# Diagonal blocks of a token ranking by six fused multiply-and-compare steps, and three pairs' late additions moved from TensorE to VectorE and GpSimd

## The reference, cut to what matters

```
ub = np.sum(np.maximum(q * k_min, q * k_max), axis=-1)      # a bound for each query and chunk
top_chunks = np.argsort(ub, axis=-1)[..., -top_k:]          # top_k = 6
scores = np.where(sel & causal, scale * q @ k.T, -1e9)
attn = exp(scores - max) / sum(exp(scores - max));  x = attn @ v
...
expert_idx = np.argmax(x @ w_gate, axis=1)
keep = np.argpartition(-gw, capacity)[:capacity]            # capacity = 80
out[tok_idx] = gate_w[tok_idx, None] * (np.maximum(x[tok_idx] @ w1[e], 0) @ w2[e])
```

## Time and profile before

| | us |
|---|---|
| median of 3 runs | 268.12 |
| lowest and highest run | 266.79, 274.02 |
| profiled execution | 266.53 |
| its span, first to last instruction | 264.8 |
| TensorE busy in the span | 256.2 |
| VectorE busy | 213.2 |
| GpSimd busy | 211.3 |
| ScalarE busy | 149.6 |

### The profile page before, as it was taken

How to read it: one execution, slowest core, us unless ns; L and a number is a source line. 1 busy time by engine, 2 the same in 40 slices (tenths; PEclk the granted TensorE clock), 3 DMA queues, 4 the chain that set the end, 5 groups by cost and what they waited for, 6 DMA issues and landing times.

```text
span 264.8 us, 9133 instructions
## 1 busy us (share of the span) xinstructions
PE 256.2 (97%) x3824; PEld 164.4 (62%) x3824; DVE 213.2 (81%) x582; ACT 149.6 (56%) x227; POOL 211.3 (80%) x280
## 2 busy tenths in 40 slices
PE   7799999999999999999999999999999999989993
PEld 7366566666666566666665666656665657676763
DVE  6886696778989988867889889899999998983332
ACT  2295656565667564647584546564856665873320
POOL 6068889998999899897989898979899971726872
PEclk9999999999999999999999999999999999999999
DMA  9989989999799989997999999999799996941782
GB/s 147 189 145 149 235 225 261 228 187 224 125 208 180 209 145 195 173 219 125 215 160 215 171 190 164 215 162 324 142 207 184 328 212 142 165 103 40 136 167 91
DMA packets 148616, 48.34 MB, mean 183 GB/s; under 512 B 131583, under 2 KB 138870, under 8 KB 148512
## 3 DMA queue, kind: packets, MB, share of 16 engines
q1 hardware_dynamic: 135504, 28.73, 54.1%
q0 software_dynamic: 9936, 18.64, 38.6%
q10 hardware_dynamic: 3136, 0.39, 1.0%
HBM read 57.03 MB, written 11.01 MB: 257 GB/s over the span
## 4 chain that ended last, share of the span: by engine, by line
PE 91%; DVE 3%; ACT 2%; DMA 1%; issue 1%; ACTq 1%; POOL 0%; DVEq 0%
PE OB L637 28%; PE SC L546 27%; PE SC L567 7%; PE OB L1395 4%; PE MM L673 4%; PE SC L1369 4%; PE MM L650 3%; PE OB L721 2%; PE MM L474 2%; PE SC L474 2%; PE MM L513 2%; DMA qn<-in_q_dram 1%; ACT EXB L576 1%; PE MM L712 1%; PE MM L982 1%
## 5 line engine op out<-in xcount | busy, mean ns | idle before, releaser
L576 ACT ACTIVATE EXB<-SC 128x1024 f32<-128x1024 f32 (+1 forms) x87 | 83.1, 966 | 35.6 <-PE SC L546 23.9
L602 POOL TENSOR_TENSOR ES<-ES,EXB 128x512 f32<-128x512 f32 (+1 forms) x81 | 84.4, 1044 | 5.1
L546 PE MATMUL SC<-qT,kT 64*128 64x512 f32 (+3 forms) x476 | 86.3, 464 | 0.1
L637 PE MATMUL OB<-EXB,vn 128*64 128x256 f32 (+3 forms) x704 | 72.9, 361 | 0.0
L637 PEld LDWEIGHTS OB<-EXB,vn 128*64 128x64 f32 x704 | 46.1, 137 | 24.0 <-issue 10.4
L546 PEld LDWEIGHTS SC<-qT,kT 64*128 64x128 f32 x476 | 39.2, 187 | 15.8 <-issue 11.5
L602 POOL TENSOR_TENSOR ES<-EXB 128x512 f32<-128x512 f32 (+1 forms) x29 | 45.3, 1561 | 2.4
L586 POOL TENSOR_SCALAR_AFFINE_SELECT EXB<-EXB 128x256 f32<-128x256 f32 x79 | 34.9, 452 | 5.0 <-ACT EXB L576 5.0
L645 ACT ACTIVATE oT<-OB 128x512 f32<-128x512 f32 (+1 forms) x32 | 15.7, 490 | 40.1 <-PE OB L637 40.1
L567 PE MATMUL SC<-unsT,ind 64*128 64x256 bf16 (+5 forms) x238 | 35.6, 295 | 0.1
L567 PEld LDWEIGHTS SC<-unsT,ind 64*128 64x128 bf16 x238 | 11.8, 95 | 15.9 <-issue 7.1
(11 more groups left out here) (270 smaller groups left out, 405.0 us busy)
## 6 DMA issues: line engine op xcount, KB each, us to landing
w1s<-in_moe_w_dram POOLq DMA_DIRECT2D x8, 1024.0 KB, 8.6
w2s<-in_moe_w_dram POOLq DMA_DIRECT2D x7, 1024.0 KB, 13.9
vn<-in_v_dram SPq DMA_DIRECT2D x32, 192.0 KB, 4.5
kn<-in_k_dram SPq DMA_DIRECT2D x62, 96.0 KB, 3.2
qn<-in_q_dram SPq DMA_DIRECT2D x62, 96.0 KB, 3.5
out_dram<-w1s SPq DMA_DIRECT2D x2, 1536.0 KB, 7.2
out_dram<-out_dram SPq DMA_DIRECT2D x2, 1536.0 KB, 9.8
x_rows<-xp SPq DMA_DIRECT2D x7, 384.0 KB, 3.9
```

The source lines that it names most:

```text
L546: op("pe", lambda: pe.matmul(o, kT[j][pr, ts(kt)], qT[j][pr, q0:q1], start=not flags and (not cols or cols[0] == 0), stop=bool(flags)), r= ...
L576: op("act", lambda: ac.activation(Ex(st, None, 0, W), src, ACTF.Exp, scale=SCALE), r=pk, w=[f"E{st}"])
L602: op(e, lambda: sy.queue[e].tensor_tensor(o, in0, in1, ALU.add), r=[f"E{s2}", f"E{first[0]}"] if first else [f"E{s2}"] + kt, w=kt)
L637: op("pe", lambda: pe.matmul(OB[pr, q0:q1], vn[s][:, kt, h, :], ex, start=(n == 0), stop=last), r=[f"vn{s}{h}", "ES0" if st is None else f ...
```

## The change

`direct` names no pair any more. So in pairs 5, 9 and 13 the eight products of line 668 are gone, VectorE makes the addition of line 608, and the second late addition is GpSimd's in pairs 5 and 9 and VectorE's (line 611) in pair 13. `rank_own` is gone, and `rank_diag` is six instructions, one per block, each of which multiplies the 128 by 128 triangle by the block's weights, one scalar for each partition, and compares the product with the block's part of G. Thirty small products are put ahead of TensorE's first ones, and of those 40 are left in place of 52; their results are not used. The instructions of the changed kernel have other line numbers: the fused ones stand in line 835, the comparisons in 842, the count in 973.

```diff
                 def direct(i):
-                    return mid(i) and i > NPB and i % NPB == 1
+                    return False
...
-                def rank_own(b):
-                    tq = bass.AP(triQ, 0, [[128, 128], [0, NT], [1, 128]])
-                    gb = bass.AP(gt6, 0, [[NT, 128], [1, NT], [0, 128]])
-                    op("dve", lambda: ve.tensor_tensor(T1v(b).rearrange("p (a b) -> p a b", a=NT), tq, gb, ALU.mult),
-                       r=["triQ", "gt6"], w=["T1"] + Ck(b, NT - 1))
-
                 def rank_diag(b):
-                    for j0, n in ((NT - 1, 1), (0, NT - 1)):
-                        o = Cs(b, j0, n, 0, 128)
-                        a = T1v(b)[:, j0 * 128:(j0 + n) * 128].rearrange("p (a b) -> p a b", a=n)
-                        g = G[:, S + j0 * 128:S + (j0 + n) * 128].rearrange("p (a b) -> p a b", a=n)
-                        op("dve", lambda: ve.tensor_tensor(o, a, g, ALU.is_ge), r=["T1", "grow"] + Ck(b, NT - 1),
-                           w=[f"D{jt}" for jt in range(j0, j0 + n)] + Ck(b, j0))
+                    for jt in range(NT):
+                        op("dve", lambda: ve.scalar_tensor_tensor(Cs(b, jt, 1, 0, 128)[:, 0, :], triQ[:], gt6[:, jt:jt + 1], G[:, S + jt * 128:S + (jt + 1) * 128],
+                                                                  ALU.mult, ALU.is_ge), r=["triQ", "gt6", "grow"], w=[f"D{jt}"] + Ck(b, jt))
...
-                warm(52, 152)
+                for n in range(30):
+                    c = n % 4 * 32
+                    op("pe", lambda: pe.matmul(SC[1][c:c + 32, 0:32], ident_f[:, 0:32], ident_f[:, 0:32], start=True, stop=True),
+                       r=["ident_f"], w=["SC1"], inc=False)
+                warm(40, 152)
...
-                    if live and kk == 0:
-                        rank_own(bb)
```

## The result

The changed kernel takes 282.01 us (median of 6 runs, 279.80 to 285.37) against 268.97 for the kernel before (median of 6, 266.79 to 274.02): a ratio of 1.049, 95% interval 1.042 to 1.056. The prediction had 276.0 and a range up to 277.8. So the sign was right, the loss of 13.0 us was half as large again as the 8.5 forecast, and the time is outside the range.

The account below looks back on a forecast made before the run. It took TensorE, busy 97% of the span, as the bound. Later count starts in pairs 6, 10 and 14 of 2.4 + 2.4 + 3.7 = 8.5 us, on a base of 267.5, gave 276.0, range 270.5 to 277.8.

Parts of the forecast that it names:

- the sums of pairs 5 and 9: TensorE's sums there wait for GpSimd's extra late addition: a loss of 0.41 us each instead of a saving.
- VectorE's lateness behind it: VectorE some 0.6 us late behind the count, taken as 0; 0.6 for each of three, 1.8, kept for the range.
- The start costs 0: Thirty small products (1.7 us) and 40 others (4.1) end at 7.3, hidden before the first useful product at 8.61.
- the rule of the Trainium skill: Two-SBUF-input VectorE instructions contend with SBUF-reading GpSimd ones, second issued blocked: loss 8.5 us with it, 0.9 without.
- the price of an undisturbed fused instruction: VectorE's diagonal blocks: taken as 0.29 us, between 0.21 and 0.44, plus 0.03 between two.
- the order of the turns: Pair 5's comparisons: addition of 768 runs before comparison 3, the last ends at 97.20, and the count starts 2.4 us later.
- the first order that the forecast gives: Pair 13: addition of 768 goes before comparison 1, addition of 512 before comparison 3; comparisons end at 208.5, count 3.7 later.
- the base: Time of the kernel before, taken as 267.5 us, the middle of the four executions known.
- Free fused instructions: Rival, 0.11: fused instructions take no turns with GpSimd; only 0.41 us in pairs 5 and 9 is lost, 268.4.
- only one short addition: Rival, 0.12: only one short addition stands before the last comparison; 3 us lost in all, 270.5.
- only TensorE's work: Rival, 0.04: 0.67 us less TensorE work and no new wait, 266.8.
- the slow start: Rival, 0.03: TensorE's first useful products run at 1.2 GHz, some 2 us taking 4; 278 with the forecast.

Follow-up runs that it names:

- 13 idle products: The changed kernel with 13 TensorE products of unused results ahead of the count in pairs 6, 10 and 14: 281.41 us, ratio 1.048.
- one early: The changed kernel with the first of the six fused instructions put ahead of the sums at the start of the same pair: 276.44 us, ratio 1.025.
- folds only: The kernel before with only `direct` changed, so the late additions return to VectorE and GpSimd; old diagonal comparisons and start kept: 273.42 us, ratio 1.019.
- fused only: The kernel before with the new six-instruction `rank_diag` and without `rank_own`; late additions and start as before: 274.15 us, ratio 1.021.
- 13 and 24 idle products: The changed kernel with unused TensorE products ahead of the count, 13 in pairs 6 and 10, 24 in pair 14: 282.09 us, ratio 1.052.
- addition held back: The changed kernel with GpSimd's addition of 768 in pairs 6, 10 and 14 also waiting for the last comparison: 273.31 us, ratio 1.019.
- four early: The changed kernel with the first four of the six fused instructions ahead of the sums at the start of the same pair: 268.17 us, ratio 1.001.

## Why the prediction was right and wrong

**Right.** The products of line 668 are gone and the sums of pairs 5 and 9 start 0.40 later against their pair's begin (0.41 forecast); in pair 13 they start where they did (211.69 against 201.68, less the shift of 10.04). The fused instructions beside GpSimd's additions take 0.82 and 0.77 (0.8). Comparisons of nearly 2 us lie behind the addition of 768. TensorE waits at the count in the three pairs, and VectorE's lateness behind it is worth 0 in pair 6: in the kernel with 13 idle products line 513 comes 7.78 us behind the count's block 4, against 7.76 before. The start costs 0:

```profile
1.54 1.07 PE L1086 MATMUL SC<-ident_f 128*32 128x32 f32 x60 [1.54 <-DVE ident_f L387]
2.54 5.04 PE L1070 MATMUL SC<-ident_bf 128*128 128x152 bf16 x40
8.62 0.51 PE L474 MATMUL MM<-qT,kmm 64*32 64x160 f32 x16 [1.04 <-DVE kmm L458]
```

The useful products start at 8.62, against 8.61. The terms inside this 0 were off and made up for each other: the thirty small products took 1.07 (1.7 forecast) and the 40 took 5.04 (4.1), and the last of them ends 1.04 ahead of the useful ones. The trace agrees with the rule of the Trainium skill that the prediction weighed (SBUF — State Buffer, Who interferes with whom) where the fused instruction of 0.82 was issued at 90.50, behind the addition of 90.37. It does not agree on who is blocked where the two are issued almost together. The sixth fused instruction of pair 13 was issued at 213.60, GpSimd's addition of 768 at 213.62, and the addition still ran first; with one early, a comparison issued at 207.78 ran behind an addition issued at 207.80. Both times an instruction of VectorE was still running, and GpSimd had the next turn.

**The step that failed** is the price of an undisturbed fused instruction, taken as 0.29 (and 0.03 between two) from between 0.21 and 0.44, and with it the order of the turns that the forecast drew from it. The price is 0.352, and 0.035 between two. Over three that is 0.2, and the comparisons began at 93.61, not at 93.41. By then the first select had had its turn ahead of the last fused instruction and the second had it ahead of the first comparison, and the addition of 768, issued at 94.03, came ahead of the second comparison instead of the third; this left the fourth to the addition of 512. So the last comparison ended at 98.40, not at 97.20, and the count started 3.60 later in place of 2.4. In pair 13 the forecast had all six fused ones ahead of the addition of 768, at about 203.7 (its own terms, six at 0.32 and two selects of 0.26 from 201.61 on, add up to 204.05); the sixth was issued just ahead of the addition and still had its turn behind it, a second addition of 512 came in, and the count started 4.93 later in place of 3.7. One early shows the size of this step: with 0.4 us less ahead of them, the four comparisons of pair 5 take 3.78, which is the length forecast (93.41 to 97.20), and in pair 13 no fused instruction lies behind the addition of 768, the first comparison does, as in the first order that the forecast gives, and the count starts 3.68 later. The place where it flips was not measured more closely than between starts of 93.21 and 93.61.

That makes 12.1 instead of 8.5, and 267.5 + 12.1 = 279.6 is outside the range by itself. Of the 6.0 us between 276.0 and 282.01 it is 3.6. Another 1.5 is the base: the forecast took the kernel before as 267.5, and its median over six runs is 268.97. That leaves 0.9 in the medians for a term that the sum did not have: around the waits the granted clock falls to 0.50, which costs up to 5.4 us in a profile in which all three places show it. The prediction had a rival with the lower rate, but at the start of the kernel.

**The other rivals.** Free fused instructions, or only one short addition, are refuted by the rows above, "only TensorE's work" by the table, and the slow start by the useful products at 8.62 and the periods ahead of pair 6, which are those of before.

## What to carry to other kernels

Where two engines take turns instruction by instruction, an added instruction costs what the other engine puts in between, not its own time: moving one of 0.35 us took 1.4 us off the last comparison, and moving four into a stretch where VectorE stood idle removed a loss of 13 us with no work saved. So look for the place before the price, and when a forecast hangs on which of two instructions is issued first, give both orders as ends of the range. And a long wait of the matrix engine can cost more than its length: in the profile the waits of 3.0 to 3.9 us cost another 1.3 to 2.4 each, through the products at the lower clock behind them. In the medians, filling these waits won nothing back.

## What the runs showed of the hardware

That a wait costs more than its length was not expected. The granted clock went to 0.50 (1.2 GHz) around waits of TensorE of 3.0, 3.0 and 3.9 us (the changed kernel), 3.5 (one early, pair 14), 1.85 (13 idle products, pair 14), 1.74 (folds only, pair 14), 1.89 (fused only, ahead of the table) and 1.7 us (13 and 24 idle products, last stage). In some places it fell within the wait and in others behind its end, with products already under way again. It stayed at 1.00 in pair 6 with waits of 0.68 (addition held back), 1.11 (folds only), 1.40 (fused only) and 1.46 us (one early).

The length of a wait alone does not decide. At the start, ahead of line 474, TensorE stands 2.1 us with four early and 2.2 with 13 and 24 idle products, and the clock stays at 1.00 in both. The window of the second has the same columns as those above:

```profile
6.00:9.00 3.00, 0.77 (x27) 1.00 0.89 141
```

The Trainium skill (TensorE: Matmul & The Clock Gate, Part 1) says that an idle TensorE is gated down to 1.2 GHz and is given 2.4 GHz again by sustained work. The two levels are those of the rows, and the idle products show that without the standing the clock stays up at the counts; why some waits bring it down and others of like length do not stays open.
